# Expert 0's second tile: its token cast made right behind the first tile's, on VectorE

## The reference

```
logits = x @ w_gate;  expert_idx = argmax(logits);  gate_w = probs[i, expert_idx]
disp[e, pos] = x[i]                       # at most capacity tokens for each expert
h = maximum(einsum('ecd,edf->ecf', disp, w1), 0.0)
y = einsum('ecf,efd->ecd', h, w2)
out[i] = gate_w[i] * y[expert_idx[i], pos[i]]
```

## Time and profile before

| what | value |
|---|---|
| median of 3 runs | 416.16 us (416.16, 416.44, 414.52) |
| profiled execution, own time | 414.46 us |
| its span, first to last instruction | 412.7 us |
| granted TensorE clock, mean | 0.997 |
| TensorE busy | 401.9 us, 97% |
| VectorE, ScalarE, GpSimd busy | 61%, 46%, 57% |

### The profile page before, as it was taken

How to read it: one execution, slowest core, us unless ns; L and a number is a source line. 1 busy time by engine, 2 the same in 40 slices (tenths; PEclk the granted TensorE clock), 3 DMA queues, 4 the chain that set the end, 5 groups by cost and what they waited for, 6 DMA issues and landing times.

```text
span 412.7 us, 9450 instructions
## 1 busy us (share of the span) xinstructions
PE 401.9 (97%) x3655; PEld 386.0 (94%) x3655; DVE 250.5 (61%) x583; ACT 188.3 (46%) x409; POOL 234.1 (57%) x239
## 2 busy tenths in 40 slices
PE   8999999999999999999999999999889999999995
PEld 7799799999999999999999999998889999999995
DVE  7787955376566546654663487775567466475532
ACT  4786553233433333333343455443446465465520
POOL 3789865567865785578334335166072744746531
PEclk9999999999999999999999999999999999999998
DMA  7999996213130303020009001833767758668100
GB/s 279 404 395 348 349 373 248 75 46 111 49 119 2 139 21 119 2 87 21 2 2 361 3 2 38 302 102 67 307 191 220 248 175 307 183 201 270 69 33 28
DMA packets 26442, 64.99 MB, mean 157 GB/s; under 512 B 11787, under 2 KB 19509, under 8 KB 24224
## 3 DMA queue, kind: packets, MB, share of 16 engines
q1 hardware_dynamic: 24464, 59.68, 42.0%
q0 software_dynamic: 1792, 4.73, 3.0%
q10 hardware_dynamic: 144, 0.00, 0.0%
HBM read 51.98 MB, written 13.21 MB: 158 GB/s over the span
## 4 chain that ended last, share of the span: by engine, by line
PE 84%; DVE 6%; issue 4%; DMA 2%; ACT 2%; POOL 1%; SPq 0%; POOLq 0%; DVEq 0%; ACTq 0%
PE bank L1423 24%; PE bank L1425 24%; PE bank L1424 24%; PE bank L1444 2%; DMA we_raw<-wexp 2%; PE bank L1473 1%; PE bank L1509 1%; PE bank L1513 1%; PE bank L1502 1%; PE bank L1505 1%; DVE we_lo L1363 1%; PE bank L1600 1%; PE bank L1774 1%; PE bank L1686 1%; PE bank L1775 1%
## 5 line engine op out<-in xcount | busy, mean ns | idle before, releaser
L730 POOL TENSOR_TENSOR g_lo<-elu,g_hi 128x256 fp32r<-128x256 f32 x95 | 73.8, 778 | 87.2 <-ACT g_hi L913 86.6
L1423 PE MATMUL bank<-xt,wd_hi 128*128 128x256 f32 x285 | 80.5, 283 | 0.6 <-DVE elu L1228 0.6
L1425 PE MATMUL bank<-xt,wd_lo 128*128 128x256 f32 x285 | 80.4, 282 | 0.0
L1424 PE MATMUL bank<-xt,wd_hi 128*128 128x256 f32 x285 | 80.3, 282 | 0.0
L904 ACT ACTIVATE elu<-elu 128x256 f32<-128x256 f32 x96 | 40.1, 418 | 75.6 <-DVE elu L1220 75.1
L1423 PE MATMUL bank<-wd_hi,g_hi 128*128 128x392 f32 (+1 forms) x192 | 67.4, 351 | 0.0
L1425 PE MATMUL bank<-wd_hi,g_lo 128*128 128x392 f32 (+1 forms) x192 | 65.2, 340 | 0.0
L1228 DVE SCALAR_TENSOR_TENSOR elu<-elu,bank 128x256 f32<-128x256 f32 x96 | 40.2, 419 | 41.1 <-ACT elu L904 41.1
L1424 PE MATMUL bank<-wd_lo,g_hi 128*128 128x392 f32 (+1 forms) x192 | 65.1, 339 | 0.0
L913 ACT CAST g_hi<-elu 128x256 fp32r<-128x256 f32 x96 | 39.0, 406 | 44.0 <-DVE elu L1228 44.0
L1423 PEld LDWEIGHTS bank<-xt,wd_hi 128*128 128x128 f32 x285 | 53.9, 189 | 1.3 <-DVE elu L1228 1.1
(11 more groups left out here) (221 smaller groups left out, 947.8 us busy)
## 6 DMA issues: line engine op xcount, KB each, us to landing
we_raw<-wexp SPq DMA_DIRECT2D x8, 1536.0 KB, 9.0
wd_raw<-wexp SPq DMA_DIRECT2D x8, 1536.0 KB, 6.5
rkt<-rkt SPq DMA_DIRECT2D x12, 512.0 KB, 5.7
nat<-nat SPq DMA_DIRECT2D x9, 672.0 KB, 5.2
wd_raw<-win SPq DMA_DIRECT2D x4, 768.0 KB, 8.6
wd_raw<-wout SPq DMA_DIRECT2D x4, 768.0 KB, 8.9
wo_tr<-wouttr SPq DMA_DIRECT2D x1, 3072.0 KB, 17.5
slots<-blank SPq DMA_DIRECT2D x1, 2702.0 KB, 14.1
```

The source lines that it names most:

```text
L730: nc.gpsimd.tensor_tensor(g_lo[:, f % 4, :], elu[:, f % 2, :], g_hi[:, f % 4, :].bitcast(F32), ALU.subtract).then_inc(s_glo, 1)
L1423: mm(dst, w_hi, x_hi, start=start, stop=False)
L1424: mm(dst, w_hi, x_lo, start=False, stop=False)
L1425: return mm(dst, w_lo, x_hi, start=False, stop=stop)
```

## The change

VectorE's cast of the second tile's tokens, with the semaphore step of s_tok[0] that it carries, moves from behind tile 1's hidden rows and expert 1's rows to right behind the first tile's cast. In the program it passes two subtractions for expert 1's w1 (L1316), gated(0), expert_cols(0, 1), tile_row, two tile_lo and expert_x(0, 1). Nothing is added or left out.

```
@@ -1310,6 +1310,7 @@
             link(V.tensor_tensor(gt[0][:, 1, :], gt[0][:, 1, :], ps_s[1][:, 0:2], ALU.add))
             tile_lo(1, ps_ht[0], s_aghi, s_aglo, 1)
             tokens_of(0, s_atok)
+            tokens_of(1, s_tok[0])
             for c in range(N1 - 1):
                 dve.wait_ge(s_ehi[1], c + 1)
                 cols = slice(c * ECH, (c + 1) * ECH)
@@ -1378,7 +1379,6 @@
             for b in range(2):
                 tile_lo(b, ps_ht[1], s_gehi, s_gelo, ET // 2)
             expert_x(0, 1)
-            tokens_of(1, s_tok[0])
             link(V.tensor_copy(part3[:, 0, :], ps_tot))
             link(V.tensor_tensor(part3[:, 1, 0:1], part3[:, 0, 0:1], early0[:, :], ALU.subtract))
             link(V.tensor_tensor(part3[:, 1, 1:2], part3[:, 1, 0:1], early0[:, :], ALU.max))
```

## The result

| what | before | after |
|---|---|---|
| median | 415.35 us (6 runs, 414.52 to 416.44) | 411.62 us (6 runs, 411.03 to 411.75) |
| profiled execution, own time | 414.46 us | 411.03 us |
| its span | 412.7 us | 409.3 us |

The ratio is 0.9916, with a 95% interval of 0.9899 to 0.9932: 3.5 us faster, between 2.8 and 4.2. The forecast was 413.3 us in a range of 411.2 to 415.5, a gain of 2.9.

The account below looks back on a forecast made before the run. TensorE, busy 97% of the span, was taken as the bound, with idle time only in expert 1's window. 0 + 0 - 2.86 us took the profiled 414.46 to 411.6 and the median 416.16 to 413.3, range 411.2 to 415.5.

Parts of the forecast that it names:

- The bound and the chain: TensorE, busy 97%, bounds; only expert 1's window has idle pieces, traced to the late token cast and expert 2's w1 load.
- (1): The cast leaving its old place, between expert_x and the small chain for n_over: worth nothing.
- (2): The cast at its new place shifts VectorE by 0.06 to 0.14 us, covered by 1.24 idle before hrow: cost 0.
- (3): SyncE passes its token wait earlier; expert 2's w1 load goes out at about 281.6, 6.0 us before 287.63.
- (4): Expert 2's w1 lands in time: ScalarE's 4.1 us wait goes, with 1.9 to 3.1 us to spare.
- (5): TensorE in expert 1: steps follow at 2.10 us each, expert 2 starts at 301.98 instead of 304.84, gain 2.86.
- (6): Idle piece before expert 2 goes: VectorE's third w1 subtraction leads GpSimd's by 0.4 us; otherwise 0.6 is lost.
- (7): After expert 1: later experts stay at 16.80 us, the gain reaches the end; loop entry costs 0, at most 1.05.
- A: Rival: the cast costs VectorE its place before GpSimd at 274, hrow 1.85 us later; net gain 1.0, 415.2; chance 0.09.
- B: Rival: part of the idle time stays, from the lost subtraction turn or loop entry; gain 1.2 to 2.3; chance 0.18.
- C: Rival: no gain, as w1 isn't the last wait and ScalarE finds another; 416.2 us; chance 0.06.
- D: Rival: slower, as load_x(2, 0) follows at once on load_x(1, 1) and delays its landing; 418.3 us; chance 0.04.

Follow-up runs that it names:

- E2: Kernel before, with the second token cast also made early without a signal and repeated in its old place with it: 414.38 us (before 414.45), ratio 0.9996.
- E1: Kernel before, both token casts in place, only their two semaphores exchanged so SyncE is told early: 411.28 us (before 414.45), ratio 0.9925.
- E3: Kernel before, with the late token cast put in front of expert_x(0, 1), its signal 0.95 us earlier: 413.29 us (before 414.45), ratio 0.9978.
- E6: Kernel before, with the late token cast between tile 1's two tile_lo, signal about 2.5 us earlier: 412.43 us (before 414.85), ratio 0.9947.
- E9: The kernel before, unchanged, profiled once more: 415.30 us in the profiled execution, 0.84 more than the first profile.
- E11: Kernel before, GpSimd's first w2 subtraction for expert 2 made to wait for VectorE's third w1 subtraction, right count: 413.62 us (before 414.75), ratio 0.9981.
- E4: Kernel before plus a GpSimd wait whose count was reached in expert 0, so it never held: 414.81 us (before 414.45), ratio 1.0006; profiled 412.36.
- E10: Kernel before with the GpSimd wait that never held, profiled once more: 414.32 us in the profiled execution.
- E12: Changed kernel plus two small linked VectorE reductions behind the two token casts: 414.24 us (before 414.75), ratio 0.9985.
- E5: Changed kernel plus three small linked VectorE copies behind the two token casts: 417.0 us (before 414.85), ratio 1.0052.
- E7: Kernel before, with the late token cast behind gated(1)'s wait for TensorE, signal about 2.1 us later: 417.05 us (before 414.85), ratio 1.0075.
- E8: Changed kernel with the copy of n_seen made by a reduction in place of a cast: 410.98 us (before 414.85), ratio 0.9913.

## Why the prediction was right

*The bound and the chain* were right: only expert 1's window changed, and in the profiled pair by 17.72 - 14.87 = 2.85 us for a forecast of 2.86. The times of the two profiled executions differ by 3.43; 0.48 of that is the earlier start of expert 1.

*(1), (2), the cast itself*: worth nothing (E2), 0.07 us of shift, under VectorE's idle time of 1.15 before hrow.

*(3), the signal*: it alone gives the gain (E1). SyncE then waited for TensorE's s_he, and the load went out at 281.08, 0.5 before the forecast, all of it the earlier start of this execution.

*(4), the landing*: ScalarE waited no more. The landing of w1 itself is not in the changed kernel's trace, but its data had all been moved by 287.1, 6.0 us after the issue (1.57 MB on the hardware queue since 281.08). The w2 issued at 286.97, as large, landed in 6.7, inside the 6.3 to 6.9 that I took. In the kernels with a later signal w1 took 6.8 to 8.5 (E3, E6, E9, E11), more than the 7.49 that I took as the long case. What makes it take longer is not shown; the same kernel had 7.5 and 8.2 (E9).

*(5), (6), both idle pieces*: gone, and VectorE was in front by 0.34 where I had 0.4. That the second piece is VectorE's turn is shown by E4 against E10, two executions of one kernel, with the kernel before and E2 on E10's side. E11's median gain agrees, while its one profile can't show it, as the clock fell in it. In E3's profile the turn was won and in E6's, with an earlier signal, it was lost: a signal that is early, but not enough, leaves this piece to chance. Nothing like "one us for each us" holds between the signal and the time.

*(7)*: later experts stayed at 16.80, and the loop's entry cost nothing.

*The sum's footing* was the part that I mis-sized. I wrote 411.6 on the profiled footing (411.03 came) and 413.3 on the median's (411.62 came), as I took the median's distance from the profile, 1.7, for a constant of the kernel. It is not. That median was of three executions, and two of them (416.16 and 416.44) are the highest of this kernel on record. The 62 executions that ran beside E1 to E12 have a median of 414.5, the profile's own time, and 414.5 - 2.86 is 411.6, the changed kernel's median. So mechanism and size were right, the forecast stood 1.7 too high by a draw of three, and the measured median lies near the low end of the range, 411.2.

What the kernel before scatters by (412.4 to 416.4) is shown in part. In six profiles with the signal late, w1 reached ScalarE 7.3 to 8.5 us after its issue, the turn was won or lost (1.2), and the clock fell or not (1.7 by itself, 0.1 on top of a lost turn); the cast near 83.4 adds its 0.5. Falls are few: of the 62 executions six have a mean granted clock of 0.996 or lower; E9 and E11, where the clock fell, have 0.993 and 0.994. In the changed kernel's profile none of the first three reaches TensorE, its runs lie within 0.7 us, and its median stands 0.6 over its profile, which had the cast near 83.4 free. Whether its mean gain is over the 2.85 of the pair isn't shown: it is 3.5 by the ratio (2.8 to 4.2) and 3.1 in E1 (2.2 to 4.1).

*Rivals.* A: the margin of 0.26 held (0.20 left). The Trainium skill, "SBUF — State Buffer", section "Who interferes with whom", says that issue order decides who blocks. E12 and E5 agree: VectorE's two subtractions take 4.57 when the first is in front of GpSimd's and 6.64 and 6.69 when it is behind. The loss I gave A (1.85) is between what E12 shows in its profiled execution (1.1) and in its median (2.9). B, C and D did not come; D's slip of load_x(1, 1) isn't there, as the transposition begins at 278.55, directly behind gated(0).

## What to carry over

When an engine waits for a load, look at what stands in front of the load's issue in the queue program: here a small signal that the load didn't need held back a later wait that was met 6 us before the load went out, and the signal's place on VectorE decided it. Count a removed wait not only by its length in one profile but by what it triggers in other executions: a lost turn against GpSimd and a fall of TensorE's clock both hung on the time of one landing. And where two engines come within a few tenths of a microsecond of each other, a median of three runs is a draw of lots: here it stood 1.7 over that of 62. Take more runs and a second profile of the kernel before, and don't add the distance between a median and a profile to a forecast as if it were a constant.

## What the runs showed of the hardware

- TensorE's clock fell from 2.4 to 1.2 GHz (granted clock 1.00 to 0.50) soon after idle pieces of 1.83 us (E9) and 2.15 (E11), and before the end of pieces of 3.70 (E7) and 4.25 (E5). It did not after 1.14 (before), 1.45 (E10) and, in one execution, 1.92 (E12). What decides between 1.83 and 1.92 isn't shown. Beside the idle time a fall cost 1.7 us in E11, and in E5 2.3: from tile 1's second transposes to expert 1's first matmul it took 7.26 there and 4.93 in E12's profile.
- A VectorE copy of 2 elements per partition, begun 0.20 behind a GpSimd subtraction, was held for the rest of it: 2.26 us, where the two same copies in front took 0.16 and 0.17 (E5). The cast of L1142, 0.02 to 0.03 behind another, took 0.74 in nine profiles and 0.16 in four, and as a reduction 0.15 in the one profile of it (E8). The Trainium skill, "SBUF — State Buffer", section "Who interferes with whom", says that copies and casts can take the pair of ports that is shared with GpSimd and that a reduction on this chip never does; these rows agree, the last one for one execution.
- The same 1536 KB load was taken up by ScalarE, where that was waiting for it, between 6.8 us (E3) and 8.5 us (E11) after its issue, and in two executions of one kernel 7.5 and 8.2 us after it (before, E9). The cause of the spread isn't shown.
